# Fused attention and two MLPs on one Trainium2 core: gate product kept in PSUM, output lag two, turned rows beside the scores, statistics by pairs

## The reference

```
scores = q @ k.T / 8                                  # 4 batches x 8 heads, 576 x 576, head dim 64
scores = where(scores >= max(scores) - tau, scores, -1e9)
attn   = exp(scores - max) / (sum + 1e-9) @ v         # [4, 8, 576, 64]
x = attn as [2304 tokens, 512]
x = (s * relu(x @ w_in)**2 + b) @ w_out               # layer 0, d_ff 2048
h = x @ w2_in;  out = (h * sigmoid(1.702 * h)) @ w2_out   # layer 1
```

## Time and profile before

| | us |
|---|---|
| median of 3 runs (lowest, highest) | 1111.01 (1108.86, 1111.34) |
| the profiled execution: its time | 1111.1 |
| its span, first to last instruction | 1109.3 |
| PE busy, share of the span | 1043.1, 94% |
| POOL busy | 779.7, 70% |
| ACT busy | 673.2, 61% |
| DVE busy | 608.1, 55% |
| granted TensorE clock, mean | 0.984 |

### The profile page before, as it was taken

One profiled execution on the slowest core, in us unless ns is written; L12 is line 12 of the kernel. 1 busy time (PEld: TensorE's weight loads), 2 busy tenths in 40 slices (PEclk: granted clock), 3 DMA queues, 4 the chain that ended last, 5 costly groups with the idle time before them and its releaser, 6 DMA issues.

```text
span 1109.3 us, 18120 instructions
## 1 busy us (share of the span) xinstructions
PE 1043.1 (94%) x5904; PEld 920.0 (83%) x5904; DVE 608.1 (55%) x1544; ACT 673.2 (61%) x1255; POOL 779.7 (70%) x773
## 2 busy tenths in 40 slices
PE   4878589999999899999999999999999999999998
PEld 3666478888888788887989989889999998999997
DVE  5899989998999899893222232322222223222222
ACT  4677466777677667765676666645545445454543
POOL 4666588888788778874666756667667667676673
PEclk9899799999999999999999999999999999999999
DMA  4122577777678776676333333333534444344431
GB/s 137 44 89 77 135 183 196 211 207 213 171 201 215 181 196 183 174 189 170 122 115 123 125 120 126 121 121 111 170 124 153 132 138 138 126 155 128 151 126 66
DMA packets 126621, 162.63 MB, mean 147 GB/s; under 512 B 27328, under 2 KB 68928, under 8 KB 126528
## 3 DMA queue, kind: packets, MB, share of 16 engines
q1 hardware_dynamic: 126528, 161.47, 49.6%
HBM read 124.85 MB, written 4.72 MB: 117 GB/s over the span
## 4 chain that ended last, share of the span: by engine, by line
PE 74%; DVE 16%; issue 3%; SPq 3%; POOL 1%; DMA 1%; ACT 1%; DVEq 0%; ACTq 0%; POOLq 0%
PE y_ps L449 31%; PE scores L431 25%; PE shared L431 6%; DVE scores L504 6%; PE scores L343 5%; PE scores L396 5%; DVE prob L528 4%; DVE blocks L543 3%; SPq L273 2%; PE shared L396 1%; DMA raw_out<-slabs_a 1%; DVE limit L511 1%; DVE gate L557 1%; PE shared L458 1%; POOL k_lo L788 1%
## 5 line engine op out<-in xcount | busy, mean ns | idle before, releaser
L808 POOL TENSOR_TENSOR win_lo<-raw_in,win_hi 128x512 fp32r<-128x512 f32 x192 | 288.6, 1503 | 96.6 <-ACT win_hi L669 96.5
L815 POOL TENSOR_TENSOR wout_lo<-raw_out,wout_hi 128x512 fp32r<-128x512 f32 x192 | 253.3, 1319 | 101.8 <-ACT wout_hi L676 101.8
L557 DVE TENSOR_TENSOR gate<-scores,gate 128x384 f32<-128x384 f32 x134 | 74.7, 558 | 409.0 <-ACT gate L686 298.2
L449 PE MATMUL y_ps<-wout_lo,g_hi 128*128 128x512 f32 x576 | 227.9, 396 | 0.0
L449 PE MATMUL y_ps<-wout_hi,g_hi 128*128 128x512 f32 x576 | 227.7, 395 | 0.0
L449 PE MATMUL y_ps<-wout_hi,g_lo 128*128 128x512 f32 x576 | 227.7, 395 | 0.0
L704 ACT CAST g_hi<-gate 128x384 fp32r<-128x384 f32 x192 | 98.6, 514 | 139.3 <-PE y_ps L449 138.4
L431 PE MATMUL scores<-act_hi,win_lo 128*128 128x384 f32 x536 | 180.9, 337 | 0.0
L431 PE MATMUL scores<-act_hi,win_hi 128*128 128x384 f32 x536 | 180.5, 337 | 0.0
L431 PE MATMUL scores<-act_lo,win_hi 128*128 128x384 f32 x536 | 180.0, 336 | 0.0
L637 ACT ACTIVATE prob<-scores,neg_max 128x576 f32<-128x576 f32 (+2 forms) x160 | 118.5, 741 | 92.4 <-DVE scores L504 81.8
(11 more groups left out here) (66 smaller groups left out, 1645.8 us busy)
## 6 DMA issues: line engine op xcount, KB each, us to landing
raw_in<-slabs_a SPq DMA_DIRECT2D x96, 256.0 KB, 3.0
raw_out<-slabs_a SPq DMA_DIRECT2D x96, 256.0 KB, 2.9
raw_in<-slabs_b SPq DMA_DIRECT2D x96, 256.0 KB, 2.6
raw_out<-slabs_b SPq DMA_DIRECT2D x96, 256.0 KB, 2.6
qk_raw<-qk SPq DMA_DIRECT2D x32, 576.0 KB, 4.1
prob_t<-blocks SPq DMA_DIRECT2D x144, 100.0 KB, 2.9
prob_t<-blocks SPq DMA_DIRECT2D x144, 80.0 KB, 2.6
v_sb<-v SPq DMA_DIRECT2D x16, 320.0 KB, 3.2
```

The source lines that it names most:

```text
L449: mm = nc.tensor.matmul(y_ps[g][:], gp[:, n % 2, toks], wp[n % RING_OUT][:], start=(f == 0 and k == 0), stop=(f == SLABS - 1 and k == 2))
L808: nc.gpsimd.tensor_tensor(win_lo[n % RING_IN][:], raw_in[:, n % 2, :], win_hi[n % RING_IN][:].bitcast(F32), ALU.subtract).then_inc(win_lo_ ...
L815: nc.gpsimd.tensor_tensor(wout_lo[n % RING_OUT][:], raw_out[:, n % 2, :], wout_hi[n % RING_OUT][:].bitcast(F32), ALU.subtract).then_inc(wo ...
```

## The change

- `gated` writes its product back into the PSUM bank of hidden, in layer 0 with the factor s. `gated_hi` reads it there, in layer 0 with the bias b, and `gated_lo` reads it there too. `affine` is gone. A bank of hidden is free only when `gated_lo` has read it.
- OUT_LAG is 2. ACT does gate, (copy of rows), both weight casts and `gated_hi` of the same step, in `step(s)`; DVE does `gated(s)` and `gated_lo(s)` in beat s.
- In riding beats turned rows go two 128 x 128 blocks at a time into a spare part of `scores[0]`, ahead of the beat's scores, in six beats a tile, without the bank `shared`.
- Raw weights are loaded into the buffer in which POOL then writes the low part; rings are 4 and 5 deep, and loads are issued one step earlier. They wait for the product that last read the buffer.
- Limit, sum + eps and inversion are made once per beat on two columns; `add_eps` goes from POOL to DVE. DVE fills the statistics once at the start.

The core of the diff, shifted left where it is indented; on the order of PE's and ACT's lists only the new lines are shown:

```diff
-OUT_LAG = 3
-RING_IN, RING_OUT = 3, 5
+OUT_LAG = 2
+IN_HI, IN_LO, OUT_HI, OUT_LO = 3, 4, 4, 5
+IN_EARLY, OUT_EARLY = 3, 2
...
-    return (done, f) if done < LAYER_TILES and f < DC else None
+    if done >= LAYER_TILES or f >= (RIDES if s < FIRST_PURE else DC):
+        return None
+    return done, f
...
-    if n >= 2:
-        sp.wait_ge(win_lo_ready, n - 1)
+    if n >= IN_LO:
+        sp.wait_ge(h_ready, n - IN_LO + 1)
...
-    if n >= 2:
-        sp.wait_ge(wout_lo_ready, n - 1)
+    if n >= OUT_LO:
+        sp.wait_ge(y_step_done, n - OUT_LO + 1)
...
-    if 2 <= s + 1 < STEPS:
-        load_out(s + 1)
-    if 2 <= s + 2 < STEPS:
-        load_in(s + 2)
+    if OUT_EARLY <= s + 2 < STEPS:
+        load_out(s + 2)
+    if IN_EARLY <= s + 3 < STEPS:
+        load_in(s + 3)
...
-    if n < FIRST_PURE:
-        shared_free(n, turns_by(n))
+    if 0 < n < FIRST_PURE:
+        pe.wait_ge(g_lo_ready, n)
     elif n == FIRST_PURE:
         pe.wait_ge(masked, TILES)
         pe.wait_ge(context_lo_ready, len(PIECES))
+        pe.wait_ge(x_lo_ready, turns_by(n - 1))
     elif n >= FIRST_PURE + H_RING:
-        pe.wait_ge(square_ready, n - H_RING + 1)
+        pe.wait_ge(g_lo_ready, n - H_RING + 1)
...
+def turn_riding(tile, r):
     pe.wait_ge(y_copied, GROUPS * (tile + 1))
+    g, c = r // 2, r % 2 * 2
+    for half in range(2):
+        mm = nc.tensor.transpose(scores[0][:, half, HALF:HALF + P],
+                                 rows_a[:, g, (c + half) * P:(c + half + 1) * P], ident[:])
+    mm.then_inc(rows_turned, 1)
...
+    s = beat - MLP_FROM
+    j = 2 * beat
+    if j < TILES or turn_due(s) is not None:
+        buffer_free(j)
+    if turn_due(s) is not None:
+        turn_riding(*turn_due(s))
+    if j < TILES:
+        scores_of(j)
+    if 0 <= j - 4 < PE_TILES:
+        turn_tile(j - 4)
+    if j < TILES or riding(beat) is not None:
+        buffer_free(j + 1)
+    if riding(beat) is not None:
+        context_of(riding(beat))
+    if j < TILES:
+        scores_of(j + 1)
+    if 0 <= j - 3 < PE_TILES:
+        turn_tile(j - 3)
     if alone(beat) is not None:
         context_of(alone(beat))
+    mlp(s)
 for s in range(FIRST_PURE, STEPS + OUT_LAG):
+    if turn_due(s) is not None:
+        turn_rows(s, *turn_due(s))
...
+def limits_of(j):
+    r = j % STATS
+    dve.wait_ge(max_ready, j + 2)
+    nc.vector.tensor_scalar(limit[:, r:r + 2], neg_max[:, r:r + 2], tau_c, None, ALU.add
+                            ).then_inc(limit_ready, 2)
+def add_eps(j):
+    r = j % STATS
+    dve.wait_ge(masked, j + 2)
+    nc.vector.tensor_scalar(row_sum_eps[:, r:r + 2], row_sum[:, r:r + 2], eps_c, None, ALU.add
+                            ).then_inc(sum_eps_ready, 2)
...
 def gated(n):
     dve.wait_ge(gate_ready, n + 1)
-    nc.vector.tensor_tensor(gate[:, n % 2, :], h_bank(n)[:, 0:TOK], gate[:, n % 2, :],
-                            ALU.mult).then_inc(square_ready, 1)
+    h = h_bank(n)[:, 0:TOK]
+    if tile_of(n)[0] == 0:
+        nc.vector.scalar_tensor_tensor(out=h, in0=h, scalar=s_c, in1=gate[:, n % 2, :], op0=ALU.mult,
+                                       op1=ALU.mult).then_inc(square_ready, 1)
+    else:
+        nc.vector.tensor_tensor(h, h, gate[:, n % 2, :], ALU.mult).then_inc(square_ready, 1)
 def gated_lo(n):
     dve.wait_ge(g_hi_ready, n + 1)
-    nc.vector.tensor_tensor(g_lo[:, n % 2, :], gate[:, n % 2, :], g_hi[:, n % 2, :].bitcast(F32),
-                            ALU.subtract).then_inc(g_lo_ready, 1)
...
 for beat in range(BEATS):
     s = beat - MLP_FROM
-    for j in tiles_of(beat):
-        if j < TILES:
-            row_max(j)
-            limit_of(j)
-        if j % 2 == 0 and alone(beat - 1) is not None:
-            context_lo(alone(beat - 1))
-        if j % 2 == 0 and 0 <= j - 1 < TILES:
-            invert(j - 1)
-        if j % 2 == 0 and s >= 1:
-            gated(s - 1)
-    for j in tiles_of(beat):
-        if j < TILES:
-            mask(j)
-        if j % 2 == 0:
-            rows_due(s)
-        if j % 2 == 0 and s >= 2:
-            gated_lo(s - 2)
+    j = 2 * beat
+    if j < TILES:
+        row_max(j)
+    if alone(beat - 1) is not None:
+        context_lo(alone(beat - 1))
+    if j < TILES:
+        row_max(j + 1)
+        limits_of(j)
+        mask(j)
+    if turn_due(s) is not None:
+        x_lo(s)
+    if j < TILES:
+        mask(j + 1)
     if riding(beat) is not None:
         context_lo(riding(beat))
-    for j in tiles_of(beat, 2):
-        if PE_TILES <= j < TILES:
-            turn(j)
-    if 2 * beat < TILES:
-        invert(2 * beat)
-for s in range(FIRST_PURE, STEPS + OUT_LAG):
-    if s - 1 < STEPS:
-        gated(s - 1)
-    rows_due(s)
-    if s - 2 < STEPS:
-        gated_lo(s - 2)
+    if s >= 0:
+        gated(s)
+    if j < TILES:
+        add_eps(j)
+    if PE_TILES <= j - 2 < TILES:
+        turn(j - 2)
+    if j < TILES:
+        invert(j)
+    if s >= 0:
+        gated_lo(s)
+    if PE_TILES <= j - 1 < TILES:
+        turn(j - 1)
+for s in range(FIRST_PURE, STEPS):
+    if turn_due(s) is not None:
+        x_lo(s)
+    gated(s)
+    gated_lo(s)
...
-        act_eng.wait_ge(g_lo_ready, n - 1)
+        act_eng.wait_ge(square_ready, n - 1)
...
-def affine(n):
-    if tile_of(n)[0] == 0:
-        act_eng.wait_ge(square_ready, n + 1)
-        nc.scalar.activation(gate[:, n % 2, :], gate[:, n % 2, :], ACT.Identity, bias=b_c, scale=s_c
-                             ).then_inc(g_full_ready, 1)
 def gated_hi(n):
-    if tile_of(n)[0] == 0:
-        act_eng.wait_ge(g_full_ready, n + 1)
-    else:
-        act_eng.wait_ge(square_ready, n + 1)
+    act_eng.wait_ge(square_ready, n + 1)
     if n >= 2:
         act_eng.wait_ge(y_step_done, n - 1)
-    nc.scalar.copy(g_hi[:, n % 2, :], gate[:, n % 2, :]).then_inc(g_hi_ready, 1)
+    if tile_of(n)[0] == 0:
+        nc.scalar.activation(g_hi[:, n % 2, :], h_bank(n)[:, 0:TOK], ACT.Identity, bias=b_c
+                             ).then_inc(g_hi_ready, 1)
+    else:
+        nc.scalar.copy(g_hi[:, n % 2, :], h_bank(n)[:, 0:TOK]).then_inc(g_hi_ready, 1)
...
+def step(s):
     n = s - OUT_LAG
+    if 0 <= s < STEPS:
+        gate_of(s)
     if n >= 0 and n % SLABS == SLABS - 1:
         copy_rows(n)
+    if 0 <= s + 1 < STEPS:
+        slab_out_hi(s + 1)
     if 0 <= s + 2 < STEPS:
         slab_in_hi(s + 2)
+    if 0 <= s < STEPS:
+        gated_hi(s)
...
+    j = 2 * beat
     if alone(beat - 1) is not None:
         context_hi(alone(beat - 1))
+    if j < TILES:
+        exponent(j)
+    if turn_due(s) is not None:
+        x_hi(s)
+    if j < TILES:
+        exponent(j + 1)
     if riding(beat) is not None:
         context_hi(riding(beat))
+    for n in tiles_of(beat, 4):
+        if 0 <= n < PE_TILES:
+            copy_turned(n)
+    step(s)
     for h in range(1, HEADS):
         if q_split_beat(h) == beat:
             split_q(h)
         if q_split_beat(h) + 1 == beat:
             split_k(h)
 for s in range(FIRST_PURE, STEPS + OUT_LAG):
+    if turn_due(s) is not None:
+        x_hi(s)
+    step(s)
...
```

More of the change, by code:

```diff
@@ L128, in turn_due, with turns_for @@
     done, f = n // SLABS - 1, n % SLABS
-    return (done, f) if done < LAYER_TILES and f < DC else None
+    if done >= LAYER_TILES or f >= (RIDES if s < FIRST_PURE else DC):
+        return None
+    return done, f
 def turns_by(s):
     return sum(turn_due(n) is not None for n in range(s + 1))
+def turns_for(tile):
+    return sum(turn_due(n) is not None and turn_due(n)[0] <= tile for n in range(STEPS))
 def build(nc, qk, v, consts_in, ident_in, slabs_a, slabs_b, out):
@@ L212, in build @@
         context_lo_ready = sem("context_lo_ready")
[L213 to L214 removed]
+        win_loaded = [sem(f"win_loaded{n}") for n in range(IN_LO)]
+        wout_loaded = [sem(f"wout_loaded{n}") for n in range(OUT_LO)]
         win_hi_ready = sem("win_hi_ready")
@@ L302, in _ @@
             sp.dma_start(ident[:], ident_in).then_inc(ident_loaded, 16)
-            for n in range(2):
+            for n in range(IN_EARLY):
                 load_in(n)
+            for n in range(OUT_EARLY):
                 load_out(n)
@@ L462, in mlp @@
             def mlp(s):
-                due = turn_due(s)
-                if due is not None:
-                    turn_rows(*due, s)
                 if s >= OUT_LAG:
@@ L526, in mask @@
                     dve.wait_ge(context_hi_ready, riding(j // 2) + 1)
+                if j % 2 == 0 and turn_due(j // 2 - MLP_FROM) is not None:
+                    dve.wait_ge(x_hi_ready, turns_by(j // 2 - MLP_FROM))
                 p = prob[0:m, j % PROBS, :].rearrange("p (a n) -> p a n", a=2)
@@ L573, in rows_due @@
-            def rows_due(s):
-                due = turn_due(s)
-                if due is not None:
-                    x_lo(*due)
+                h, hi = h_bank(n)[:, 0:TOK], g_hi[:, n % 2, :].bitcast(F32)
+                if tile_of(n)[0] == 0:
+                    nc.vector.scalar_tensor_tensor(out=g_lo[:, n % 2, :], in0=h, scalar=b_c, in1=hi, op0=ALU.add,
```

(8 more changed lines are left out.)

160 lines of the change are left out of this document (66 added, 94 removed).

## The result

The changed kernel takes 1187.2 us (median; 1185.0 to 1188.5) against 1110.9: ratio 1.069, 95% interval 1.067 to 1.071. It is slower, as forecast, but by 76 us and not 13, and outside the range. Its profiled execution took 1185.0 us, span 1183.2, granted clock 0.972 (0.984 before).

A forecast was written before the change was run, and what follows sets the result against it. While the MLP rides on attention, DVE ends short beats and PE long ones; in the MLP alone PE is almost never idle. 1111.1 + 11.0 + 7.8 - 4.2 - 1.4 = 1124.3 us; range 1107 to 1154, its own 1113 to 1134.

The forecast's parts named there:

- rival (a): Two-column limit and eps addition on DVE wait for running POOL instructions: 1151 us (1134 to 1180); chance 0.24.
- steps 2 and 4: Riding stage +7.8 us and attention alone -1.4 us, both counting a limit and an inversion fewer per beat.
- Attention alone: The 28 beats before the MLP rides: waits behind POOL of some 0.4 us each, 11 us more.
- Step 1: MLP alone: PE waits at tile ends for row copies now queued behind ACT's gate; +11.0 us.
- Steps 2 and 3: Riding stage: DVE's product waits for its own beat's hidden product, +7.8 us; turned rows beside scores, -4.2 us.
- step 2: Riding stage: DVE waits for its own beat's hidden product; five beats 33.62 us against 32.84, +7.8 us.
- Step 2's small terms: Riding stage: product and low part +0.06 us each, ACT's Identity 0.68 us, nothing booked for reading PSUM.
- Step 4: Attention alone: a limit and an inversion fewer per beat, add_eps more, -0.05 us in 28 beats; -1.4 us.
- Rival (b): Riding stage: DVE's late product doesn't reach PE, five beats take 31.72 us, kernel 1105.3 us; chance 0.16.

The follow-up runs named there:

- x1: The changed kernel with the two-column limit made by two one-column instructions; 1129.6 us, ratio to the kernel before 1.017.
- x2: The kernel before, with its limit instruction made on two columns, the second a constant zero; 1175.2 us, ratio 1.058.
- x5: x3 with DVE's list reordered in beats with a context piece: eps addition, first turn and inversion ahead of the gate product; 1100.3 us, ratio 0.991.
- x3: x1 with the copy of a finished tile's rows put ahead of the gate in ACT's step; 1108.2 us, ratio 0.9986.
- x9: The changed kernel with each POOL weight subtraction of 512 columns cut into two of 256; 1168.4 us, ratio 1.052.
- x8: x6 with layer 1's copies placed behind both weight casts as well as the gate; 1126.2 us, ratio 1.013.
- x12: x3, but in layer 0 two copies ahead of the gate and the third behind it; 1114.3 us, ratio 1.004.
- x6: x1 with the copy of a finished tile ahead of the gate in layer 0 only; 1115.6 us, ratio 1.005.

## Why the prediction was wrong

**The step that failed is the weighing and the price of rival (a), the pair-wise statistics behind POOL.** It is what happened, and it had a chance of 0.24 and a price of 27 us; it cost 58, and the result lies above even the rival's own range (1134 to 1180). In the sum itself the failing term is the pair-wise limit of steps 2 and 4, booked as "a limit and an inversion fewer" and so as a small saving, where the pair took 1.58 us against 0.21 for a single one.

- *The chance.* "No small instruction of DVE waits now, not even among busy POOL" was true of one column and said nothing of two. By the Trainium skill (VectorE: DVE Perf Modes, What auto-detection actually checks; SBUF — State Buffer, Who interferes with whom) a tensor_scalar from SBUF to SBUF with even outermost dimensions takes a mode that uses the ports shared with GpSimd, and then one of the two engines blocks the other. The traces agree: 0.21 us for all 160 singles of x1 against a mean of 1.58 in pairs, and x2 has the same in the old kernel. That one column stays clear is shown by the runs alone. A rule that is met by the very form that a diff brings in, and that no row contradicts, should have been the forecast.
- *The price per limit.* I took POOL's busy share times half an instruction, 0.54 us, as if limits came at random times. They come just after a POOL instruction has started, in all 41 of 41, and 8 of these waited over 1.6 us: the wait is 1.37 over the 0.21, two and a half times as much.
- *The path.* Ten groups of five beats at 1.6 us gave 16; from x1 to the change the riding stage has 44.3 - 6.3 = 38.0. With 1.37 for 0.54, three on the path of each group give 41. So a count of three fits the time, and the wait was what was mis-sized; which three waits lie on the path wasn't followed.
- *Attention alone:* 11 forecast, 19.3 found (16.8 + 2.5). Two thirds of that isn't the limit's own time: 28 limits of 0.65 against 56 of 0.21 are 6.4 us more. How the rest comes about is not traced.

**The rest of the sum** is to be read in x1, which has the whole change without that lock: 1129.6 us against the forecast 1124, within its own range of 1113 to 1134.

- *Step 1* (+11.0): the stalls came as worked out, 2.04 and 1.15 against 2.18 and 1.22, but the MLP alone with the rest took 15.9 - 1.6 = +14.3. What was missing is TensorE's clock behind the three stalls of 2.04, 1.54 each, 4.6 in all; the stalls themselves, 11.9 less the 1.6 of before, came out a little under the forecast.
- *Steps 2 and 3* (+7.8 - 4.2 = +3.6): +6.3. Five riding beats took 33.96 against 33.62 (before 32.84), 3.4 us over ten groups. The turned tile's extra over the pattern is 4.8 in the first case (beats 43 to 53, 238.94 to 311.61, less twice 33.96) and 2.8 in the second (beats 61 to 68, 367.50 to 416.24, less the 46.0 of seven beats of the pattern), against 4.3; together with before (5.3 and 7.5) saved 5.2, not 4.2. That DVE's wait for the product of its own beat costs time is shown by x5. But it is not where step 2 had it: there DVE's waits in long beats were free ("PE sets the pace"), and x5 changes only long beats; of the 0.78 us that it takes off five, 0.72 are in the first long beat.
- *Step 2's small terms:* the product took 0.62, the low part 0.60 in layer 0 and 0.56 in layer 1, against 0.60 as the sum of 0.54 and 0.06; the Identity took 0.58, not 0.68. The Trainium skill's 62 cycles more for PSUM sources (VectorE: DVE Perf Modes, The TRN2 errata) don't show: 0.56 from PSUM in layer 1 stands against 0.55 from SBUF.
- *Step 4* (-1.4): -2.5, but x3 and x5, with the same work there, have +0.9 and -0.5, so it can't be told from the start's own scatter.
- *Rival (b)* is not what the change does, nor x5: five beats of x5 take 33.18, not 31.72. But with the limits' waits and the stalls gone, an order of DVE's list is what lay between the change and a gain.

## What to carry to other kernels

Merging two tiny VectorE instructions into one saved nothing here (the mask starts 0.25 us behind the first of two singles in x1, 0.26 behind a pair that is free in the changed kernel) and can change the form: the two-column addition in SBUF waited for whatever GpSimd instruction was running, and in this kernel, whose engines run in step, one was just starting each time. Before queueing anything ahead of a copy that releases TensorE, ask what that thing waits for; and price a TensorE stall of about 2 us at itself and up to 1.6 us more (the lower clock came behind 10 of 14). Test the parts of a bundle by themselves: here one line cost 58 us, one order 21, and what was left beat the old kernel once DVE's list was put in order.

## What the runs showed of the hardware that was not expected

- A two-column addition of DVE took 0.22 to 0.23 us with GpSimd idle, and up to 2.68 beside it; it can sit through two GpSimd instructions in a row (2.54 us for 1.43 and 1.28). On one column it never waited, in 160 of 160. Of a reciprocal on two columns nothing is known: it never arrived while a GpSimd instruction ran.
- TensorE's granted clock fell to the 1.2 GHz level 0.3 to 1.4 us after the end of stalls of 2.04 us (8 of 9, in the changed kernel, x1 and x9) and of 2.18 us (2 of 5, in x8), at 1.5 to 1.6 us each. After the three stalls of 1.06 us (x12) and the 20 of 1.15 (changed kernel, x1, x6, x9) it stayed at the upper level.
